# A recurrent attention with two feed-forward layers on one Trainium2 core: the read of the block inverses is issued by SyncE, and their write changes places with the block write

## What is computed

```
for t in range(S):
    y[:, :, t] = einsum('bhd,bhde->bhe', rt, state)
    Sa = einsum('bhde,bhe->bhd', state, at)
    state = state * wt[:, :, None, :] - einsum('bhd,bhe->bhde', Sa, bt)
    state = state + einsum('bhd,bhe->bhde', vt, kt)
...
x = moe2(moe(attn_out))        # two matmuls each; softmax and normalisation in the first
```

## Time and profile before

| | |
|---|---|
| time, median of 3 runs | 1060.81 us (1055.99 to 1068.70) |
| the profiled execution's own time | 1065.29 us |
| its span | 1063.5 us |
| mean granted TensorE clock | 0.941 of full speed |
| PE busy, share of the span | 924.9 us, 87% |
| DVE, ACT, POOL busy | 631.1, 478.3, 217.9 us |
| DMA traffic | 64.99 MB, of which SP's queue (q1) 60.16 MB and ACT's queue (q10) 3.15 MB |
| d_read, DMA dc<-d_scr | 12 times, 256.0 KB each |

### The profile page before, as it was taken

The page is one execution under the profiler, slowest core; times in us unless marked ns, Lnnn a source line. Parts: engine busy times, 40 slices in busy tenths (PEclk is TensorE's granted clock), DMA queues, the critical chain, the costliest instruction groups (busy, mean ns, idle before and its releaser), DMA issues.

```text
span 1063.5 us, 31728 instructions
## 1 busy us (share of the span) xinstructions
PE 924.9 (87%) x13408; PEld 873.6 (82%) x13408; DVE 631.1 (59%) x1087; ACT 478.3 (45%) x1011; POOL 217.9 (20%) x452
## 2 busy tenths in 40 slices
PE   3269696688688689788799999999999999999998
PEld 3268686687678589777789999999999999999998
DVE  8857555466456465365675665657566475655644
ACT  3246445435445455453563443535344353543533
POOL 8546623523523532400000000000000000000000
PEclk9688898898898899899899999999999999999999
DMA  5725462562473454223401000000000000000000
GB/s 154 153 41 130 103 140 69 100 148 69 103 161 92 105 123 95 49 91 97 140 14 26 1 26 26 1 25 0 25 0 25 25 0 25 0 25 5 9 14 13
DMA packets 143039, 64.99 MB, mean 61 GB/s; under 512 B 118940, under 2 KB 130076, under 8 KB 142924
## 3 DMA queue, kind: packets, MB, share of 16 engines
q1 hardware_dynamic: 93580, 60.16, 21.5%
q10 hardware_dynamic: 49344, 3.15, 3.3%
HBM read 45.98 MB, written 17.30 MB: 60 GB/s over the span
## 4 chain that ended last, share of the span: by engine, by line
PE 63%; DMA 15%; DVE 8%; ACT 6%; issue 5%; SPq 2%; POOL 0%; ACTq 0%; DVEq 0%; POOLq 0%
DMA dc<-d_scr 9%; PE acc L1116 5%; PE px L331 5%; DMA d_scr<-s_x 5%; PE acc L1117 5%; PE acc L1118 5%; PE mid L1116 3%; PE mid L1117 3%; PE mid L1118 3%; PE bank L1116 3%; PE bank L1117 3%; PE bank L1118 3%; PE pa L300 3%; PE pq L393 2%; PE pr L355 2%
## 5 line engine op out<-in xcount | busy, mean ns | idle before, releaser
L1469 DVE SCALAR_TENSOR_TENSOR stage<-mid,slopes 128x512 f32<-128x512 f32 x96 | 66.4, 691 | 107.1 <-ACT slopes L1310 107.1
L1306 ACT ACTIVATE stage<-mid 128x512 f32<-128x512 f32 x96 | 57.1, 595 | 160.2 <-PE mid L1187 160.2
L1116 PE MATMUL acc<-wo_h,act_h 128*128 128x320 f32 x384 | 121.5, 317 | 6.8 <-DVE act_l L1396 6.0
L1382 POOL TENSOR_TENSOR stats<-stats 128x1 f32<-128x1 f32 x24 | 13.2, 551 | 556.0 <-DVE stats L1444 556.0
L1117 PE MATMUL acc<-wo_h,act_l 128*128 128x320 f32 x384 | 118.5, 309 | 0.0
L1118 PE MATMUL acc<-wo_l,act_h 128*128 128x320 f32 x384 | 118.2, 308 | 0.0
L1116 PE MATMUL mid<-zT_h,w_h 128*128 128x256 f32 x384 | 108.6, 283 | 5.4 <-DVE zT_l L1396 5.4
L1117 PE MATMUL mid<-zT_h,w_l 128*128 128x256 f32 x384 | 108.2, 282 | 0.0
L1118 PE MATMUL mid<-zT_l,w_h 128*128 128x256 f32 x384 | 107.9, 281 | 0.0
L808 POOL TENSOR_TENSOR al<-al,prod 40x512 f32<-40x512 f32 x48 | 62.7, 1307 | 182.2 <-DMA al<-a_features_first 136.3
L1310 ACT ACTIVATE slopes<-stage,minus_alpha 128x256 f32<-128x256 f32 x192 | 87.4, 502 | 3.1
(11 more groups left out here) (163 smaller groups left out, 2475.0 us busy)
## 6 DMA issues: line engine op xcount, KB each, us to landing
wkb<-wkb_features_first SPq DMA_DIRECT2D x46, 242.5 KB
rvu<-rv_features_first SPq DMA_DIRECT2D x48, 160.0 KB
l_scr<-lb SPq DMA_DIRECT2D x24, 256.0 KB, 4.4
al<-a_features_first SPq DMA_DIRECT2D x48, 80.0 KB
sv<-v_time_first SPq DMA_DIRECT2D x48, 80.0 KB, 3.8
x_scr<-x SPq DMA_DIRECT2D x48, 80.0 KB
out<-y_sb SPq DMA_DIRECT2D x11, 320.0 KB, 2.3
d_scr<-s_x SPq DMA_DIRECT2D x12, 256.0 KB, 5.1
```

Of the source, the lines that this page charges most:

```text
L1116: pe.matmul(o, left[0], right[0], start=start, stop=False)
L1306: act.activation(neg[q % 2][:], mid[q % 2][:], ACT.Relu, scale=-1.0).then_inc(neg_ready, 1)
L1469: dve.scalar_tensor_tensor(out=act_f[q % 2][:], in0=mid[q % 2][:], scalar=0.0, in1=slope[q % 2][:], op0=ALU.max, op1=ALU.add).then_inc(act ...
```

## The change

`d_read` moves from ACT to SP. SP issues it in the prologue behind `d_write(0)` (ahead of `l_read(1)` and the loads of groups 5 and 6) and behind `d_write(1)` (ahead of `load_wkb(7)`), and from step 2 on in every even step up to 20, behind `l_read` and in front of `load_wkb`. Its two waits, for `spread_d` of the pair before and for the landing of `d_write`, move with it. At the end of an odd step `d_write` now stands in front of `l_write`.

```diff
 (SP, def sync)
+        def d_read(p):
+            wait(sp, dd_ready, NB * p)
+            sp.wait_ge(d_out[p % 2], use(p, 2, 16))
+            blocks = d_scr[p].rearrange("k l x -> (k l) x").rearrange("(l b) (s t) -> (b s) l t", b=2 * NB, t=SB)
+            sp.dma_start(dc[:], blocks).then_inc(d_back[p % 2], 16)
...
             d_write(0)
+            d_read(0)
             l_read(1)
...
             d_write(1)
+            d_read(1)
             load_wkb(7)
...
             if n % 2 == 0 and n + 4 < NG:
                 l_read((n + 4) // 2)
+            if n % 2 == 0 and 0 < n < NG - 2:
+                d_read(n // 2 + 1)
             if n + 8 < NG:
                 load_wkb(n + 8)
...
             beside(sp, n)
+            if n % 2 == 1 and n + 3 < NG:
+                d_write((n + 3) // 2)
             if n % 2 == 1 and n + 5 < NG:
                 l_write((n + 5) // 2)
-            if n % 2 == 1 and n + 3 < NG:
-                d_write((n + 3) // 2)
 (ACT, def scalar)
-            d_read(0)
             act.wait_ge(masks_loaded, 16)
             spread_d(0)
...
             take_uT(n)
-            if n % 2 == 0 and n + 2 < NG:
-                d_read(n // 2 + 1)
             if 0 < n and n + AHEAD - 1 < NG:
                 take_kbn(n + AHEAD - 1)
```

More of the change, by code:

```diff
@@ L710, in spread_a @@
                 act.copy(a_bd[ER[half], half], al[m % 7][ER[half], half]).then_inc(a_bd_ready, 1)
[L712 to L716, removed]
         def spread_d(p):
```

## The result

The changed kernel took 1009.47 us (median of 4 runs, 1007.43 to 1018.29) beside 1061.78 us before (4 runs, 1055.99 to 1068.70): ratio 0.9521, 95% interval 0.9439 to 0.9603. In a second measurement, on another occasion and beside seven runs of the kernel before, the ratio was 0.9456 (0.9389 to 0.9523). The profiled execution took 1018.29 us, its span is 1016.5; it is the slowest of the first four. A second execution of the same kernel was profiled as e12_change_again (1003.66 us, span 1001.9).

A forecast was written before the change was run, and what follows sets the result against it. Bound by the attention's read of the inverses, with ACT's spread_d ahead of take_rhs. Savings 36.2 + 5.9 + 1.6 = 43.7 us: profiled 1065.29 becomes 1021.6, or 1017 against the median; range 1002 to 1034, 8 in 10 for 994 to 1042.

The forecast's parts named there:

- even steps 4 to 14: Attention steps shortened to 17.1 us by an earlier, faster dc read; with step 2, 36.2 us saved.
- step 2: Even step shortened like the others, less 2.2 us once because SP waits for the late solve before the block write.
- prologue: First dc read, issued first by SP, takes 5.0 us instead of 10.89; 5.9 us saved.
- steps 16 and 18: Even steps without large loads: dc lands 12.3 us in, 0.3 and 1.3 us earlier; 1.6 us saved.
- signs of being wrong: dc still 9 us or more, block write later than 0.3 us in beyond step 2, or DVE waiting for wkb.
- The read on SP's queue: In even steps the read goes out 6.5 us in and takes 5.8 us, passing the loads behind it.
- The slower rival: SP stands before the write of the inverses, waiting for POOL's solve, and delays the block write; 1073 us, chance 0.03.
- The first rival: PE's shorter pause in even steps lets the full clock hold, saving 18.7 us more; 998 us, chance 0.18.
- What SP pays: Issuing dc holds SP up 3.2 us per even step; large loads issued by 12 us in; cost 0.
- the rival of the late loads: dc's pieces hold SP up 6 us, loads land late, 2 us of each even step return; 1031 us, chance 0.05.
- ACT's wait for dc: ACT's 56.5 us of waiting for the read of the inverses would be about halved.
- The second rival: The read takes its mean of 10.3 us on any queue; only earlier issue saves 4.9 us; 1056 us, chance 0.12.

The follow-up runs named there:

- e12_change_again: The changed kernel once more, without an edit; 1005.28 us, ratio 0.9456.
- e3_behind_loads: The changed kernel with the read issued behind the two large loads on SP's queue instead of in front of them; 1030.82 us, ratio 0.9682.
- e2_read_only: The changed kernel with the two writes back in the old order, so only the read's move to SP remains; 1014.68 us, ratio 0.9528.
- e9_act_late: The kernel before with the writes swapped and the read on ACT placed behind take_state, which waits for PE; 1082.43 us, ratio 1.0190.
- e1_swap_only: The kernel before with only d_write and l_write swapped, the read staying on ACT; 987.21 us, ratio 0.9250.
- e4_read_first: The changed kernel with the read directly behind l_write, ahead of load_a and l_read; 986.49 us, ratio 0.9248.
- e6_act_beside: The kernel before with the writes swapped and the read on ACT placed behind spread_a; 992.96 us, ratio 0.9347.

## Why the prediction was right, point by point

The forecast was 1017 us, 43.7 us saved; the profiled executions differ by 47.0 us and the medians by 52.3. Its terms, in the profiled executions:

| term | forecast | measured | in e12_change_again |
|---|---|---|---|
| even steps 4 to 14 | 32.0 us | 32.3 us | 35.9 us |
| step 2 | 4.1 us | 2.0 us | 6.1 us |
| prologue | 5.9 us | 4.7 us | 7.0 us |
| steps 16 and 18 | 1.6 us | 1.6 us | 0.8 us |
| odd steps 3 to 15 | 0 | 3.9 us | 9.1 us |
| everything behind | 0 | 2.5 us | 2.8 us |

The first term carries the forecast, and its mechanism was right. That it agrees within 0.3 us is luck: the same program gave 35.9 us in the other execution, and both savings are against one profile of the kernel before. The errors of the small terms partly cancel in the first profile; in the second, all but one are on the same side and the sum is 61.6 us. The stated range, 1002 to 1034 us, is 16 us either way of 1018, not of 1017; this changes nothing. None of its signs of being wrong appeared: the read took 5.0 to 7.4 us in steps 2 to 14, and beyond step 2 the block write was issued 0.3 us into the even steps.

**The read on SP's queue.** 5.8 us were taken from step 16 of the kernel before; the median is 5.4. The six even steps came out at 17.0 us, for 17.1. The issue came 5.9 to 7.1 us into these steps, 6.5 on average, as forecast. The reason was right as to the large loads: they had made the read long. The stated cause, that dc now passes the loads behind it, was too narrow. e3_behind_loads shows that it is nearly as short behind them; what counts is that it no longer shares the engines with them, and with the loads behind them, from a second queue.

**Step 2.** The term was mis-sized. I had the solve end as in the earlier trace rows, 1.1 us into the step. In the changed kernel POOL's last instruction starts at 103.13 and the step at 99.59:

```profile
103.13 0.85 POOL L833 TENSOR_TENSOR s_x<-s_x,masks 128x256 f32<-128x256 f32 x1
```

```profile
104.01 0.40 SPq L222 DMA_DIRECT2D d_scr<-s_x  x1
104.46 1.41 SPq L206 DMA_DIRECT2D l_scr<-lb  x2
```

The write goes out 4.4 us into the step, and the block write, 4.9 us in, pays for it: 21.4 us instead of 19.3. In e12_change_again the same write went out before its step started, and step 2 was 17.3 us long. The slower rival was thus a real mechanism, with one place and varying from run to run. A part of the late solve is one instruction: POOL's `s_t<-s_in,s_x 128x15` took 2.64 us at 100.11, and 0.21 in the kernel before and 0.22 in e12_change_again. No experiment was made on why.

**The prologue.** The read took 4.26 us, for 5.0, and landed 6.9 us earlier than before. 2.3 us of it were lost behind that. A lower clock is the likely cause, though no run changed the clock alone. The windows (us, busy of PE, PEld, DVE, ACT, POOL, granted clock, DMA share, GB/s), first of the changed kernel's profile, then of e12_change_again:

```profile
56.00:62.00 6.00, 3.76 (x119) 3.40 (x113) 5.18 (x10) 0.14 (x1) 5.06 (x13) 0.76 0.01 3
```

```profile
56.00:62.00 6.00, 3.77 (x121) 3.41 (x122) 5.79 (x11) 1.23 (x3) 5.14 (x12) 1.00 0.01 3
```

The same program in the same stretch had 0.76 of the clock in one execution and all of it in the other. solve_u of step 0 starts at 63.85 and 61.51.

**The clock.** The first rival, given 0.18, came true in part. PE's timeline of the changed kernel shows the pause in front of solve_u and how long solve_u then takes (1.93 us at 1.2 GHz, 1.13 at 2.4):

```profile
121.01 1.93 PE L365 MATMUL pr<-rhs,hh 64*64 64x40 f32 x32 [7.61 <-ACT rhs L685]
...
223.49 1.13 PE L365 MATMUL pr<-rhs,hh 64*64 64x40 f32 x32 [1.53 <-ACT rhs L685]
...
288.33 1.93 PE L365 MATMUL pr<-rhs,hh 64*64 64x40 f32 x32 [2.78 <-ACT rhs L685]
...
320.71 1.13 PE L365 MATMUL pr<-rhs,hh 64*64 64x40 f32 x32 [1.74 <-ACT rhs L685]
```

In the windows behind the third and the second of these the granted clock is 0.52 and 1.00:

```profile
288.00:295.00 7.00, 6.67 (x86) 6.25 (x88) 5.19 (x7) 3.81 (x12) 6.27 (x10) 0.52 0.58 120
223.40:228.00 4.60, 4.51 (x111) 4.31 (x113) 4.50 (x7) 3.47 (x10) 4.36 (x4) 1.00 0.33 77
```

The last one, after 1.74 us, is between: its solve_u is at full clock, and over the 6.3 us from 320.7 on the window has 0.73. solve_u alone does not tell: in e12_change_again it took 1.13 us in step 3 although PE had paused 3.52 us, and the low clock came only behind it:

```profile
114.60:118.00 3.40, 3.39 (x68) 3.28 (x69) 3.30 (x6) 1.68 (x5) 3.17 (x4) 0.70 0.36 98
```

Step 9, which began at full clock and kept it, is 13.7 us long where it had been 16.8; the forecast's 2.67 us for a held clock was 3.1 there. In e12_change_again steps 9 and 15 were 13.7 and 13.9 us long, after pauses of 1.68 and 1.61 us. The pause of some 3 us on which the rival counted was too long: after 2.78 us (above) and 3.68 us (step 11) the clock was 0.52 and 0.54. The seven odd steps 3 to 15 are 3.9 us shorter together. The clock also goes with much of the spread: of the change's eight measured runs one had a mean clock of 0.953 and took 1018.29 us, the other seven had 0.963 or 0.964 and took 1003.66 to 1011.30 us. That low-clock run is the profiled one. It lies 8.8 us above its median and the profiled execution before 3.5 above its own, which is why the medians differ by 5 us more than the profiles.

**What SP pays.** In step 2 the issue of dc takes 1.20 us and that of the large loads 2.79, and the loads are out 14.6 us into the step; in step 12 it is 11.3 us, for the 12 forecast. The dc issue and what the loads' issue takes above its 0.66 us are 3.3 us in step 2, for the 3.2 forecast. No wait of DVE for wkb appears. The cost of 0 stands, and the rival of the late loads falls. **ACT's wait for dc** was to be about halved, and went down by a third; step 2's 8.0 us is the largest part of what is left. **The second rival**, that the queue does not matter, falls with the change's own reads, with e2_read_only, and with e3_behind_loads beside e9_act_late.

**Everything behind.** Step 22 was 1.6 us longer than before, and from solve_u of step 23 (491.37 us before, 448.19 after, 43.2 earlier) to the end 3.8 us were won. 1.8 of them lie in the last chunk of the feed-forward layers. No experiment was made on this.

**What was not foreseen** is that one half of the change is better than the whole. The prediction saw that the write of the inverses would land 2 us into the step, and that l_read would be issued at 6.1, and did not ask what the 4 us between them were worth. e1_swap_only and e4_read_first answer: some 20 us. Most of it came from the even steps, which fell from 17.0 to 14.6 us and 15.1 us.

## What to carry to other kernels

In this kernel a transfer of small pieces suffered from large loads when they moved at the same time on another queue. Putting it on the queue of the loads helped, at the price of what is issued behind it, and so did giving it a start of a few us on its own queue. When a wait is moved to a queue that works in order, look at what stands in front of it there: here the read inherited the wait for the block write, and the early write of the inverses went unused until the read was placed before it. And test the halves of a change alone, since the two can work against each other.

## What the runs showed of the hardware that was not expected

- The same read of 256 KB in pieces of 64 bytes, issued some 8 us into the even step, takes 5.8 to 7.2 us on the queue that carries 485 KB of loads in front of it (e3_behind_loads, steps 2 to 14, issued 7.0 to 9.4 us in), and 8.9 to 12.4 us on the other queue beside them and the loads that follow (e9_act_late). In step 12 of the kernel before all but 152 of its 4096 packets went within 3 us, and those 152 took 4.4 us more beside the loads.
- A DMA issue on ACT left before four copies that stand ahead of it in the program had begun (e6_act_beside: issued at 229.64, copies from 229.96 to 232.0). So "works through its own in order", as the kernel is described above, does not hold for an issue and the copies ahead of it. A semaphore wait ahead did hold it back: behind `take_state` it left 8.1 to 8.5 us into the even steps (e9_act_late).
- A DMA of small pieces holds up the next issue on its queue: in e3_behind_loads the issue of `x_scr` takes 4.35 to 6.87 us behind it in steps 2 to 14, and 0.67 to 0.69 in odd steps.
- The same program had different clocks in the same stretch in two executions (0.76 and 1.00 at 56 to 62 us). In the changed kernel's first profile a pause of PE of 2.8 us was followed by the low clock, one of 1.5 us was not, and one of 1.7 us in part.
